# Four loads under way instead of three during the attention of a fused attention and two-MLP kernel, with the instruction orders rewritten to suit

## The chip, the core and the metric

The kernel runs on one core of one Trainium2 chip. A core has a matrix engine (PE; its weight loads are listed apart as PEld), a vector engine (DVE), a scalar engine (ACT), a general engine (POOL) and a sync engine (SP) that here only issues DMA transfers. Each engine works through its own list of instructions in order, and they wait for one another on semaphores. The metric is the time of the device for one execution in microseconds (us). The kernel before takes 612.75 us, the median of 3 runs (612.43 to 613.37).

## The reference

```
scores = scale * q @ k^T                 # q, k, v: 2 x 8 heads x 576 x 64, float32
mask: heads 0-3 local   (0 <= row - col < 32)
      heads 4-7 strided (col <= row, and row, col equal modulo 32)
x = softmax(scores) @ v                  # laid out as 1152 tokens x 512
h = max(x @ w_in, 0);  x = (h * h) @ w_out                       # 512 -> 2048 -> 512
p = domain_probs / (sum(domain_probs) + 1e-9)
out = sum over 4 experts e of p[:, e] * (max(x @ w1[e], 0) @ w2[e])   # 512 -> 1024 -> 512
```

## The kernel before

Every order in it is written out by hand, engine by engine.

**Attention.** The heads go in pairs, and a pair of one batch entry is a unit n = 0 to 7; units 0, 1, 4, 5 are local, the others strided. For each unit PE makes the scores (`scores(n)`: a mask product, L1313, and then the products of q and k, L1321), transposes the probabilities (`prob_transposes(n, h)`, L1334) and multiplies with v (`outputs(n)`, L1364). DVE takes the row maximum and subtracts it (`scores_max`, `scores_less`), ACT exponentiates (`exps`), DVE sums and inverts (`recip`), POOL multiplies (`normalised`, L621), ACT copies the transposed probabilities out of PSUM (`pT_copy`, L699) and then the result into `y` (`att_out`, L705). `keep_going` (L1370) gives PE idle products whose results nobody reads; `idle=` in a call says how many.

**First products.** The MLP products are done in a Strassen-like form with 7 products M1, M2, M6, M7, M4, M5, M3 in place of 8, each in three passes over a high and a low part of the numbers (L1374 to L1376). Their operands are made by `wa_high` (ACT, L717) and `wa_low` (POOL, L568) from the weights in `raw_a`; by `first_sum` (DVE) from sums of these; by `x_high` (ACT, L737) and `x_low` (POOL, L610, one of them on DVE, L955) from `y` or differences `t_form` of it; and by `wb_high` (ACT, L726) and `wb_low` from `raw_b`. `wa_high` of the first group waits until all four parts of `raw_a` are there, and the first `first_sum` too. `wb_high` waits for both parts of `raw_b`. M7 also needs `c_block(0, C11)` on DVE, which waits for the last `pT_copy`. The first of these products (block 0) lie between the last units of the attention, and after them PE goes through the rest of both MLPs.

**Loads.** SP issues them all, apart from half of one k. `load_qk(n)` is three transfers (q 288 KB, k 144 KB for each head) into one of three buffers, so it waits for `scores(n - 3)`. `load_v(n)` is 512 + 64 KB for a local unit and 384 KB for a strided one, and from n = 4 on waits for `outputs(n - 4)`. `load_a(0, parts)` brings 256 KB of weights for each part, `load_b(0, (i,))` 512 KB. Between loads stand `landed_qk(n)`, `landed_v(n)` and `landed_a(4)`, which hold SP until that load has landed, so that a fixed number of loads is under way.

Of the kernel before, what the change touches and what calls it, by code (L numbers as in the profile page):

```python
# [30 lines left out]
def attention_then_mlps(nc, qt, kt, v_near, v_last, v_far, wa, wb, probs, out):  # L31
# [60 lines left out]
    with ExitStack() as ctx:  # L92
# [313 lines left out]
        def _(sp):  # L406
# [58 lines left out]
            load_qk(2)  # L465
            landed_qk(0)
            load_a(0, (0, 1))
            landed_qk(1)
            load_v(0)
            landed_qk(2)  # L470
            load_a(0, (2, 3))
            load_qk(3)
            landed_v(0)
            load_v(1)
            landed_a(4)
            load_v(2)
            landed_qk(3)
            load_qk(4)
            landed_v(1)
            load_qk(5)  # L480
            landed_v(2)
            load_v(3)
            landed_qk(4)
            load_qk(6)
            landed_qk(5)
            load_qk(7)
            landed_v(3)
            load_v(4)
            landed_qk(6)
            load_v(7)  # L490
            landed_qk(7)
            load_v(5)
            landed_v(4)
            load_b(0, (0,))
            landed_v(7)
            load_v(6)
            landed_v(5)
# [19 lines left out]
        def _(pool):  # L517
# [109 lines left out]
            normalised(1)  # L627
            wa_low(0, A11)
            normalised(2)
            wa_low(0, A12)  # L630
            wa_low(0, S2)
            normalised(3)
            wa_low(0, S3)
            normalised(4)
            x_low(0, B11)
            normalised(5)
            x_low(0, B21)
            wa_low(0, A22)
            normalised(6)
            normalised(7)  # L640
# [3 lines left out]
            x_low(0, T1)  # L644
            x_low(0, B22)
            wa_low(0, S4)
            wb_low(0, 0)
            wb_low(0, 1)
            wb_low(0, 2)
            wb_low(0, 3)  # L650
            x_low(1, B11)
# [35 lines left out]
        def _(act):  # L687
# [86 lines left out]
            exps(1)  # L774
            pT_copy(0, 0)
            pT_copy(0, 1)
            exps(2)
            att_out(0)
            pT_copy(1, 0)
            pT_copy(1, 1)  # L780
            wa_high(0, A11)
            exps(3)
            wa_high(0, A12)
            pT_copy(2, 0)
            att_out(1)
            wa_high(0, S2)
            pT_copy(2, 1)
            x_high(0, B11)
            exps(4)
            wa_high(0, S3)  # L790
            att_out(2)
            pT_copy(3, 0)
            pT_copy(3, 1)
            wa_high(0, A22)
            exps(5)
            att_out(3)
            wa_high(0, S1)
# [3 lines left out]
            exps(6)  # L801
            pT_copy(5, 0)
            att_out(4)
            pT_copy(5, 1)
            exps(7)
            x_high(0, T2)
            first_product(0)
            att_out(5)
            x_high(0, T3)
            pT_copy(6, 0)  # L810
            pT_copy(6, 1)
            x_high(0, T4)
            pT_copy(7, 0)
            x_high(0, T1)
            pT_copy(7, 1)
            att_out(6)
            rectified(0, C11)
            wb_high(0, 0)
            x_high(0, B22)
            x_high(1, B11)  # L820
            wa_high(0, S4)
# [3 lines left out]
            rectified(0, C21)  # L825
            squared(0, C21)
            h_high(0, C21)
            wb_high(0, 2)
            wb_high(0, 3)
            rectified(0, C22)  # L830
            squared(0, C22)
# [746 lines left out]
```

## Time and profile before

| | us |
|---|---|
| median of 3 runs | 612.75 |
| profiled execution | 612.54 |
| its span in the trace | 610.7 |
| PE busy | 602.6 (99%) |
| DVE busy | 366.5 (60%) |
| POOL busy | 279.3 (46%) |
| ACT busy | 221.7 (36%) |

The span runs from the first to the last instruction; 1.84 us lie around it. PE is busy nearly throughout, but idle products count as busy too. In the chain that ended last, 94% of the span is PE, 3% DMA and 1% each SP's issues and DVE. In the span in 40 slices of 15.3 us, the DMA engines are busy 70% of the first slice, 90% of the second and 50% of the third, and 30% or less of each slice after that.

### The profile page before, as it was taken

To read this page: it belongs to the slowest core of one execution; us is meant where nothing else is said; L and a number is where in the kernel's file an instruction comes from. 1 tells how busy PE (TensorE), PEld (TensorE's weight loads), DVE (VectorE), ACT (ScalarE), POOL (GpSimd) and SP (SyncE) were. 2 spreads that over 40 slices of the span, in tenths; PEclk is the share of its full clock that TensorE was granted. 3 is DMA by queue.
4 is the path that set the end of the run, shared out by engine and by line. 5 is a ranking of instruction groups with operands and counts; after the bars stand their busy time and mean duration, and the time that the engine had idled before them with its cause. 6 is when DMAs were issued, how large, how long until landed. Compare 5 with 4: busy or idle time off the path is not lost.

```text
span 610.7 us, 11302 instructions
## 1 busy us (share of the span) xinstructions
PE 602.6 (99%) x4347; PEld 561.8 (92%) x4347; DVE 366.5 (60%) x797; ACT 221.7 (36%) x508; POOL 279.3 (46%) x230
## 2 busy tenths in 40 slices
PE   7899999999999999999999999999999999999998
PEld 6789999999999999998988989989989989989987
DVE  6787595746847878735636536636536446446452
ACT  2688373514524645511511421422332322232210
POOL 4679844551560587961560451462443353350300
PEclk9999999999999999999999999999999999999999
DMA  7953020220110220120220110220120030010012
GB/s 254 288 171 139 1 70 2 70 70 2 69 70 2 70 70 0 71 70 1 70 69 1 70 69 1 70 71 0 65 75 1 25 114 1 7 64 1 1 52 104
DMA packets 16677, 36.92 MB, mean 60 GB/s; under 512 B 2032, under 2 KB 2800, under 8 KB 16624
## 3 DMA queue, kind: packets, MB, share of 16 engines
q1 hardware_dynamic: 16544, 36.05, 17.3%
q8 instruction: 35, 0.57, 0.4%
q10 hardware_dynamic: 80, 0.15, 0.1%
q14 instruction: 18, 0.15, 0.1%
HBM read 33.84 MB, written 2.36 MB: 59 GB/s over the span
## 4 chain that ended last, share of the span: by engine, by line
PE 94%; DMA 3%; SPq 1%; DVE 1%; issue 0%; POOL 0%; ACT 0%; ACTq 0%
PE ps L1374 31%; PE ps L1376 31%; PE ps L1375 31%; DMA k_buf<-in_k 3%; PE ps L1364 1%; PE ps L1321 0%; DVE k_buf L1127 0%; PE ps L1334 0%; SPq L419 0%; SPq L412 0%; POOL prob L621 0%; SPq L438 0%; DVE ssum L919 0%; ACT y L705 0%; DVE t_form L944 0%
## 5 line engine op out<-in xcount | busy, mean ns | idle before, releaser
L1374 PE MATMUL ps<-xf_hi,wa_hi 128*128 128x288 f32 x672 | 199.3, 297 | 0.0
L1375 PE MATMUL ps<-xf_lo,wa_hi 128*128 128x288 f32 x672 | 198.3, 295 | 0.0
L1376 PE MATMUL ps<-xf_hi,wa_lo 128*128 128x288 f32 x672 | 197.6, 294 | 0.0
L574 POOL TENSOR_TENSOR wb_lo<-raw_b,wb_hi 128x512 fp32r<-128x512 f32 x48 | 61.0, 1307 | 175.9 <-ACT wb_hi L726 175.9
L1374 PEld LDWEIGHTS ps<-xf_hi,wa_hi 128*128 128x128 f32 x672 | 126.0, 187 | 0.9 <-ACT wa_hi L717 0.2
L1375 PEld LDWEIGHTS ps<-xf_lo,wa_hi 128*128 128x128 f32 x672 | 126.1, 188 | 0.5
L1376 PEld LDWEIGHTS ps<-xf_hi,wa_lo 128*128 128x128 f32 x672 | 126.5, 188 | 0.0
L1376 PE MATMUL ps<-wb_hi,h_lo 128*128 128x512 f32 (+1 forms) x292 | 113.0, 387 | 0.0
L1375 PE MATMUL ps<-wb_lo,h_hi 128*128 128x512 f32 (+1 forms) x292 | 113.0, 387 | 0.0
L1374 PE MATMUL ps<-wb_hi,h_hi 128*128 128x512 f32 (+1 forms) x292 | 112.8, 386 | 0.0
L1118 DVE SCALAR_TENSOR_TENSOR y<-ps,p_norm,y 128x512 f32<-128x512 f32 (+1 forms) x64 | 47.5, 742 | 102.3 <-PE ps L1376 102.3
L766 ACT ACTIVATE h_hi<-ps 128x288 fp32r<-128x288 f32 x128 | 50.5, 409 | 101.0 <-DVE ps L1077 100.8
L744 ACT ACTIVATE m<-ps 128x288 f32<-128x288 f32 x48 | 19.4, 413 | 183.7 <-PE ps L1376 183.7
L1374 PE MATMUL ps<-h_hi,wb_hi 128*128 128x288 f32 (+1 forms) x224 | 69.9, 312 | 0.0
L1376 PE MATMUL ps<-h_hi,wb_lo 128*128 128x288 f32 (+1 forms) x224 | 69.8, 312 | 0.0
L1375 PE MATMUL ps<-h_lo,wb_hi 128*128 128x288 f32 (+1 forms) x224 | 69.8, 311 | 0.0
L568 POOL TENSOR_TENSOR wa_lo<-raw_a,wa_hi 128x512 fp32r<-128x512 f32 x36 | 46.8, 1306 | 45.6 <-ACT wa_hi L717 45.6
L1077 DVE TENSOR_TENSOR ps<-ps,u 128x288 f32<-128x288 f32 x144 | 65.9, 459 | 2.0 <-PE ps L1376 0.3
L1376 PEld LDWEIGHTS ps<-wb_hi,h_lo 128*128 128x128 f32 x292 | 54.8, 188 | 11.1
L1375 PEld LDWEIGHTS ps<-wb_lo,h_hi 128*128 128x128 f32 x292 | 54.8, 188 | 10.9
L1374 PEld LDWEIGHTS ps<-wb_hi,h_hi 128*128 128x128 f32 x292 | 54.9, 188 | 10.8
L568 POOL TENSOR_TENSOR wa_lo<-s_form,wa_hi 128x512 fp32r<-128x512 f32 x48 | 61.3, 1296 | 7.6 <-ACT wa_hi L717 7.4
(88 smaller groups left out, 759.7 us busy)
## 6 DMA issues: line engine op xcount, KB each, us to landing
raw_a<-in_wa SPq DMA_DIRECT2D x48, 256.0 KB, 3.5
raw_b<-in_wb SPq DMA_DIRECT2D x24, 512.0 KB, 4.0
q_buf<-in_q SPq DMA_DIRECT2D x8, 288.0 KB, 4.4
k_buf<-in_k SPq DMA_DIRECT2D x15, 144.0 KB, 3.9
v_loc<-in_v_near SPq DMA_DIRECT2D x4, 512.0 KB, 4.3
result<-y SPq DMA_DIRECT2D x8, 256.0 KB, 2.0
v_str<-in_v_far SPq DMA_DIRECT2D x4, 384.0 KB, 4.4
v_loc<-in_v_last SPq DMA_DIRECT2D x4, 64.0 KB, 5.3
```

What stands on the lines that cost most here:

```text
L568: nc.gpsimd.tensor_tensor(wa_lo[:, k, :, :], where[:, i, :, :], wa_hi[:, k, :, :].bitcast(F32), ALU.subtract).then_inc(s_wa_lo, 1)
L574: nc.gpsimd.tensor_tensor(wb_lo[:, :, cols], raw_b[:, :, cols], wb_hi[:, :, cols].bitcast(F32), ALU.subtract).then_inc(s_wb_lo, 1)
L744: nc.scalar.activation(m1[:, u, :], ps[:, bank(t, M1, u), 0:HT], ACT.Copy).then_inc(s_m1, 1)
L766: nc.scalar.activation(dst, src, ACT.Relu).then_inc(s_h_hi, 1)
L1077: nc.vector.tensor_tensor(ps[:, hbank(t, q, u), 0:HT], ps[:, bank(t, k, u), 0:HT], other[:, u, :], ALU.add)\
L1118: nc.vector.scalar_tensor_tensor(out=out_acc[:, i, d], in0=src, scalar=p_norm[:, i, e:e + 1], in1=out_acc[:, i, d], op0=ALU.mult, op1=ALU. ...
L1364: ins = nc.tensor.matmul(dst, vals, probT[rows, n % 2, h, at:at + qw], start=True, stop=True)
L1374: nc.tensor.matmul(dst, a_hi, b_hi, start=first, stop=False)
L1375: nc.tensor.matmul(dst, a_hi, b_lo, start=False, stop=False)
L1376: return nc.tensor.matmul(dst, a_lo, b_hi, start=False, stop=last)
```

## The change

The order of the loads stays as it is. What moves is the wait before each: each stands one load later, so four loads are under way in place of three, and one wait (`landed_v(5)`) is gone. The orders of ACT, DVE, POOL and PE in the attention and the first MLP block are rewritten, and the idle products before `scores(4)` are gone. Nothing is computed otherwise. All lines behind the loads stand one line higher in the new file.

```
 sync:
             load_qk(2)
+            load_a(0, (0, 1))
             landed_qk(0)
-            load_a(0, (0, 1))
+            load_v(0)
             landed_qk(1)
-            load_v(0)
+            load_a(0, (2, 3))
             landed_qk(2)
-            load_a(0, (2, 3))
             load_qk(3)
+            load_v(1)
             landed_v(0)
-            load_v(1)
+            load_v(2)
             landed_a(4)
-            load_v(2)
+            load_qk(4)
...
 tensor:
             prob_transposes(0, 1)
-            outputs(0)
             prob_transposes(1, 0)
             prob_transposes(1, 1)
+            outputs(0)
             scores(3, idle=2)
             outputs(1)
             prob_transposes(2, 0)
             prob_transposes(2, 1)
-            scores(4, idle=3)
-            outputs(2)
+            scores(4)
             scores(5)
             prob_transposes(3, 0)
             prob_transposes(3, 1)
+            outputs(2)
             scores(6)
...
             product(0, M1, [1])
+            prob_transposes(6, 0)
+            prob_transposes(6, 1)
             outputs(5)
             product(0, M2, [0])
-            prob_transposes(6, 0)
-            prob_transposes(6, 1)
             product(0, M2, [1])
...
 gpsimd:
             normalised(1)
+            normalised(2)
             wa_low(0, A11)
-            normalised(2)
             wa_low(0, A12)
...
             x_low(0, T1)
+            wa_low(0, S4)
             x_low(0, B22)
-            wa_low(0, S4)
...
 vector:
             scores_max(1)
+            scores_less(1)
             recip(0)
-            scores_less(1)
+            recip(1)
             scores_max(2)
-            recip(1)
+            first_sum(S1)
             scores_less(2)
-            first_sum(S1)
+            first_sum(S3)
             recip(2)
+            first_sum(S2)
             pair_t1(0)
...
```

SP, from the loads of unit 4 on: the difference of the two orders. `v_str` and `v_loc` are v of strided and local units; `s_k_in0` to `s_k_in2` count landings in the three q and k buffers, `s_v_in0` to `s_v_in3` those of the v buffers, `s_pv` the finished `outputs`.

```order
-L431 DMA v_str<-in_v_far 128x768 [waits s_pv,s_k_in0,s_q_in0]
-L427 DMA v_loc<-in_v_near 128x2x512 [waits s_pv,s_k_in1,s_q_in1]
+L431 DMA v_str<-in_v_far 128x768 [waits s_pv,s_v_in3]
+L427 DMA v_loc<-in_v_near 128x2x512 [waits s_pv,s_k_in0,s_q_in0]
 L428 DMA v_loc<-in_v_last 64x2x128
-L445 DMA raw_b<-in_wb 128x1024 [waits s_v_in0]
-L431 DMA v_str<-in_v_far 128x768 [waits s_pv,s_v_in3]
-L445 DMA raw_b<-in_wb 128x1024 [waits s_v_in1]
+L445 DMA raw_b<-in_wb 128x1024 [waits s_k_in1,s_q_in1]
+L431 DMA v_str<-in_v_far 128x768 [waits s_pv,s_v_in0]
+L445 DMA raw_b<-in_wb 128x1024 [waits s_v_in3]
```

The second half of `raw_b` waited for v of unit 5, issued two transfers ahead of it; now it waits for v of unit 7, which is issued earlier still.

ACT at the start of the attention, from the first two `exps` (L691) on, before:

```order
4 L691 ACTIVATE raw_prob<-raw_prob 128x10x64 [waits s_less] x2
5 L699 ACTIVATE probT<-ps 128x320 [waits s_pT_ps] x2
6 L691 ACTIVATE raw_prob<-raw_prob 128x12x54 [waits s_less]
7 L705 ACTIVATE y<-ps 128x576 [waits s_pv]
8 L699 ACTIVATE probT<-ps 128x320 [waits s_pT_ps] x2
9 L717 ACTIVATE wa_hi<-raw_a 128x512 [waits s_raw_a]
```

and now (each line number is one lower):

```order
4 L690 ACTIVATE raw_prob<-raw_prob 128x10x64 [waits s_less] x2
5 L716 ACTIVATE wa_hi<-raw_a 128x512 [waits s_raw_a]
6 L698 ACTIVATE probT<-ps 128x320 [waits s_pT_ps]
7 L716 ACTIVATE wa_hi<-raw_a 128x512 [waits s_raw_a]
8 L698 ACTIVATE probT<-ps 128x320 [waits s_pT_ps]
9 L690 ACTIVATE raw_prob<-raw_prob 128x12x54 [waits s_less]
```

Two `wa_high`, with their wait for the weights, now stand ahead of the first and the second `pT_copy`, where one stood behind the fourth.

ACT around the last units, from `first_product` (L744, in the new file L743) on, before:

```order
35 L744 ACTIVATE m_62<-ps 128x288 [waits s_m] x2
36 L705 ACTIVATE y<-ps 128x576 [waits s_pv]
37 L737 ACTIVATE xf_hi<-t_form 128x576 [waits s_t0]
38 L699 ACTIVATE probT<-ps 128x384 [waits s_pT_ps,s_pv] x2
39 L737 ACTIVATE xf_hi<-t_form 128x576 [waits s_t0]
40 L699 ACTIVATE probT<-ps 128x384 [waits s_pT_ps,s_pv]
```

and now:

```order
36 L743 ACTIVATE m_62<-ps 128x288 [waits s_m] x2
37 L698 ACTIVATE probT<-ps 128x384 [waits s_pT_ps,s_pv] x2
38 L704 ACTIVATE y<-ps 128x576 [waits s_pv]
39 L725 ACTIVATE wb_hi<-raw_b 128x4x128 [waits s_raw_b]
40 L736 ACTIVATE xf_hi<-t_form 128x576 [waits s_t0] x2
41 L698 ACTIVATE probT<-ps 128x384 [waits s_pT_ps,s_pv] x2
```

The first `wb_high`, with its wait for both parts of `raw_b`, stood six rows further back; now it is ahead of the `x_high` of T3 and T4 and of the last two `pT_copy`.

## Rows read from the trace of the kernel before

**Rows 1.** PE over its first 52 us: start, length, engine, line, operation, count, [idle before <- releaser].
```profile
15.07 1.35 PE L1364 MATMUL ps<-probT,v_loc 64*64 64x32 f32 x72 [0.62 <-ACT probT L699]
...
16.99 0.71 PE L1370 MATMUL ps<-ones 128*128 128x512 f32 x2
...
17.94 1.26 PE L1321 MATMUL ps<-k_buf,q_buf 128*54 128x108 f32 x22
19.13 1.35 PE L1364 MATMUL ps<-probT,v_loc 64*64 64x32 f32 x72
21.03 0.85 PE L1334 MATMUL ps<-ident,prob 128*128 128x128 f32 x6 [0.54 <-POOL prob L621]
21.63 0.94 PE L1370 MATMUL ps<-ones 128*128 128x512 f32 x3
22.40 0.45 PE L1313 MATMUL ps<-mask_local,across 128*128 128x512 f32 x2
...
29.32 1.23 PE L1321 MATMUL ps<-k_buf,q_buf 128*54 128x108 f32 x22 [1.35 <-DMA k_buf<-in_k]
...
37.60 1.35 PE L1364 MATMUL ps<-probT,v_loc 64*64 64x32 f32 x72 [0.26 <-DMA v_loc<-in_v_last]
...
41.55 0.93 PE L1334 MATMUL ps<-ident,prob 128*128 128x128 f32 x6 [0.16 <-POOL prob L621]
...
50.77 0.30 PE L1374 MATMUL ps<-xf_hi,wa_hi 128*128 128x288 f32 x1
```
**Rows 2.** All waits of PE from 41 us to the end: us in total, times, longest.
```profile
PE ps L1334 <- POOL prob L621: 0.2, 1, 0.2
```
**Rows 3.** PE's granted clock, the span in 40 slices, in tenths (9 is 90% or more).
```profile
PEclk9999999999999999999999999999999999999999
```
**Rows 4.** The wait for the weights, seen on DVE (columns as in rows 1).
```profile
15.63 0.69 DVE L963 TENSOR_TENSOR s_form<-raw_a 128x512 f32<-128x512 f32 x1 [0.62 <-DMA raw_a<-in_wa]
```
**Rows 5.** SP's issues: start, length, line, transfer, count.
```profile
7.43 0.58 SPq L427 DMA_DIRECT2D v_loc<-in_v_near  x1
...
8.91 0.89 SPq L438 DMA_DIRECT2D raw_a<-in_wa  x2
...
31.48 0.33 SPq L431 DMA_DIRECT2D v_str<-in_v_far  x1
...
37.58 0.33 SPq L445 DMA_DIRECT2D raw_b<-in_wb  x1
```
**Rows 6.** Stretches: length, engines' busy us (count), PE clock, DMA share, GB/s.
```profile
8.00:10.50 2.50, 2.38 (x42) 1.87 (x41) 2.45 (x4) 0.74 (x1) 0.00 (x0) 1.00 0.67 199
10.50:29.00 18.50, 16.21 (x350) 13.52 (x349) 14.80 (x25) 10.85 (x22) 10.63 (x9) 1.00 0.94 298
28.00:29.00 1.00, 0.00 (x0) 0.00 (x0) 0.96 (x2) 1.00 (x3) 1.00 (x2) 1.00 0.93 195
32.50:40.50 8.00, 7.74 (x197) 7.33 (x198) 7.73 (x12) 6.02 (x14) 6.29 (x5) 1.00 0.88 291
```
**Rows 7.** ACT: columns as in rows 1.
```profile
21.64 0.61 ACT L717 ACTIVATE wa_hi<-raw_a 128x512 fp32r<-128x512 f32 x1
22.16 0.47 ACT L699 ACTIVATE probT<-ps 128x384 f32<-128x384 f32 x1
22.53 0.64 ACT L705 ACTIVATE y<-ps 128x576 f32<-128x576 f32 x1
...
40.30 0.69 ACT L737 ACTIVATE xf_hi<-t_form 128x576 fp32r<-128x576 f32 x1 [0.65 <-DVE t_form L944]
```
**Rows 8.** The chain that ended last: start, length, what.
```profile
23.65 5.53 DMA k_buf<-in_k
```
**Rows 9.** DMA issues between 37.5 and 37.9 us: count, KB each, us from issue to landing.
```profile
raw_b<-in_wb SPq DMA_DIRECT2D x1, 512.0 KB, 4.8
```
**Rows 10.** POOL: columns as in rows 1.
```profile
42.17 1.41 POOL L610 TENSOR_TENSOR xf_lo<-t_form,xf_hi 128x576 fp32r<-128x576 f32 x1 [0.76 <-DVE xf_lo L955]
...
48.97 1.29 POOL L568 TENSOR_TENSOR wa_lo<-s_form,wa_hi 128x512 fp32r<-128x512 f32 x1
```

More of the change, by code:

```diff
@@ L627, in _ @@
             normalised(1)
+            normalised(2)
             wa_low(0, A11)
-            normalised(2)
             wa_low(0, A12)
@@ L644, in _ @@
             x_low(0, T1)
+            wa_low(0, S4)
             x_low(0, B22)
-            wa_low(0, S4)
             wb_low(0, 0)
@@ L649, in _ @@
             wb_low(0, 2)
+            x_low(1, B11)
             wb_low(0, 3)
-            x_low(1, B11)
             x_low(1, B21)
@@ L774, in _ @@
             exps(1)
+            wa_high(0, A11)
             pT_copy(0, 0)
+            wa_high(0, A12)
             pT_copy(0, 1)
             exps(2)
+            pT_copy(1, 0)
             att_out(0)
-            pT_copy(1, 0)
+            wa_high(0, S2)
             pT_copy(1, 1)
-            wa_high(0, A11)
+            att_out(1)
             exps(3)
-            wa_high(0, A12)
             pT_copy(2, 0)
-            att_out(1)
-            wa_high(0, S2)
+            wa_high(0, S3)
             pT_copy(2, 1)
             x_high(0, B11)
+            wa_high(0, A22)
             exps(4)
-            wa_high(0, S3)
-            att_out(2)
             pT_copy(3, 0)
             pT_copy(3, 1)
-            wa_high(0, A22)
+            att_out(2)
             exps(5)
             att_out(3)
-            wa_high(0, S1)
             pT_copy(4, 0)
@@ L801, in _ @@
             exps(6)
+            x_high(0, T2)
+            att_out(4)
+            wa_high(0, S1)
             pT_copy(5, 0)
-            att_out(4)
             pT_copy(5, 1)
             exps(7)
-            x_high(0, T2)
             first_product(0)
-            att_out(5)
-            x_high(0, T3)
             pT_copy(6, 0)
             pT_copy(6, 1)
+            att_out(5)
+            wb_high(0, 0)
+            x_high(0, T3)
             x_high(0, T4)
             pT_copy(7, 0)
-            x_high(0, T1)
             pT_copy(7, 1)
             att_out(6)
+            x_high(0, T1)
             rectified(0, C11)
-            wb_high(0, 0)
+            wa_high(0, S4)
             x_high(0, B22)
             x_high(1, B11)
-            wa_high(0, S4)
             h_high(0, C11)
@@ L827, in _ @@
             h_high(0, C21)
+            x_high(1, B21)
             wb_high(0, 2)
-            wb_high(0, 3)
+            x_high(1, T2)
             rectified(0, C22)
             squared(0, C22)
-            x_high(1, B21)
+            wb_high(0, 3)
             h_high(0, C22)
@@ L836, in _ @@
             h_high(0, C12)
-            x_high(1, T2)
             x_high(1, T3)
@@ L1161, in _ @@
             recip(6)
+            t_forms(0, T4)
+            pair_t1(4)
             scores_less(7)
[L1163 to L1164 removed]
+            t_forms(0, T3)
             recip(7)
[L1166 removed]
             pair_t1(5)
@@ L1466, in _ @@
             prob_transposes(0, 1)
-            outputs(0)
             prob_transposes(1, 0)
             prob_transposes(1, 1)
+            outputs(0)
             scores(3, idle=2)
@@ L1473, in _ @@
             prob_transposes(2, 1)
-            scores(4, idle=3)
-            outputs(2)
+            scores(4)
             scores(5)
@@ L1478, in _ @@
             prob_transposes(3, 1)
+            outputs(2)
             scores(6)
```

72 lines of the change are left out of this document (34 added, 38 removed).

## The prediction

> **What bounds the kernel now.** I read the waits of PE first, since PE is busy 99% of the span. From 41 us to the end there is one wait, of 0.2 us [rows 2]. So 569 us of the span are PE's own work, the change touches none of it in length, and what it can bring is only how early PE gets there. Then I read PE's timeline up to that point [rows 1] for what is not needed work. It waits 0.62 us at 15.07 for ACT's copy of the transposed probabilities, 0.54 at 21.03 for POOL's probabilities, 1.35 at 29.32 for k of unit 6, 0.26 at 37.60 for v of unit 5 and 0.16 at 41.55 for POOL again. Between 21.63 and 22.40 it runs the three idle products ahead of `scores(4)`: 0.77 us. Third, what is behind the 1.35: k of unit 6 was issued at 23.65 and took 5.53 us [rows 8]. In the DMA engines' shares of the stretches [rows 6] the reader is to see that they are not idle in that time: 0.94 busy from 10.5 to 29 us, and only 0.67 from 8 to 10.5 us. A fourth load under way can fill 0.33 x 2.5 = 0.83 us of the one and 0.06 x 18.5 = 1.1 us of the other, 1.9 us in all.
>
> **The loads.** Nothing is added or removed but one wait; every load can be issued one landing earlier. The weights `raw_a`: their third and fourth part go out at 8.91 and about 9.35 [rows 5]; DVE is released by them at 15.63 after 0.62 us of waiting [rows 4]. The wait ahead of them is now that for unit 1, which was over at 7.43, where it released v of unit 0 [rows 5]; that load now goes out ahead of it. So they go out at about 7.6, some 1.25 us earlier. They can't land sooner by more than the idle share in front of them, 0.83 us; from below, they may gain nothing. I take nearly all of it, since that stretch is the emptiest: landing at 14.7 in place of 15.55 (between 14.3, the whole lead in issue, and 15.55).
>
> K of unit 6 can be issued once `scores(3)` is done. If the loads gain their whole 1.9 us, it lands at 29.18 - 1.9 = 27.3; with nothing, at 29.18.
>
> **The start of the attention: a loss.** ACT now waits for all of `raw_a` ahead of its first `pT_copy`. With R the landing, one `wa_high` takes 0.52 from start to next start, a `pT_copy` 0.37 and 0.47 to its end [rows 7]. The first copy starts at R + 0.52, the second `wa_high` at R + 0.89, the second copy at R + 1.41 and ends at R + 1.88. The second half of the transposes of unit 1 waits for that copy, takes half of 0.60 (from 21.03 to 21.63), and `outputs(0)` follows. Together `outputs(0)` and the transposes took 16.99 - 15.07 = 1.92; without the first half of the transposes, now done in the wait, 1.62. So PE has both behind it at R + 3.5 = 18.2, against 16.99: 1.2 us late, though both probabilities are ready sooner. `scores(3)` starts at 17.94 + 1.2 = 19.15.
>
> **From there to `scores(6)`: a gain.** In the run before these starts lie 29.32 - 17.94 = 11.38 us apart. Out of it go the idle products (0.77), the wait for `prob` with its small gap (21.03 - 19.13 - 1.29 = 0.6, taking 1.29 as the pitch of an `outputs` of 72 products, their 1.35 less the overlap) and the wait for k (1.35). The wait for `prob` goes because `normalised(2)` no longer has a `wa_low` of 1.29 us [rows 10] in front of it, and because transposes of unit 2 come later now. `outputs(2)` moves behind two `scores`, which gives its copies time. That leaves 8.65 us: `scores(6)` at 27.8 in place of 29.32, 1.5 us sooner. K of unit 6 has to be there by 27.8: 1.4 us of the 1.9 that the idle shares allow. `scores(3)` ends at about 20.4, the second half of k goes out within a microsecond of it, and even with the 5.53 us of before it lands at 26.9, so the buffer is not what holds it.
>
> **From `scores(6)` to the dense part.** The work is the same. The 0.26 and 0.16 may go: the transposes of unit 6 (0.6 us) now stand ahead of `outputs(5)`, which hides the landing of v, and `normalised(6)` no longer stands behind an `x_low`. Between 0 and 0.4; I take 0.2. Sum for PE: 1.7 us.
>
> **The end of the hand-over: raw_b.** ACT's first `wb_high` now stands ahead of `x_high` of T3 and T4, and it waits for the second half of `raw_b`. Before, that half went out at 37.58 [rows 5] and landed 4.8 us later [rows 9], at 42.4. POOL started on T3 at 42.17 and had the last operand of product M3 at 48.97 + 1.29 = 50.26 [rows 10]; M3 began at 50.77 [rows 1]. So POOL had 0.5 us to spare. Call the landing L: T3's `x_high` starts at L + 0.5 and takes 0.69 [rows 7], POOL starts at L + 1.2, and M3 can start at L + 1.2 + (50.26 - 42.17) = L + 9.3. To be 1.7 us sooner M3 needs L of 39.8 or less. Now that half waits for v of unit 7, which was issued at 31.48 [rows 5] as soon as `outputs(3)` was done, 1.6 us sooner now: 29.9. The DMA engines moved 291 GB/s at 0.88 from 32.5 to 40.5 [rows 6] for v7, v5, b0, v6 and b1; at 0.94 that is 7.5 us. With 1.0 us from issue to first bytes (31.48 to 32.5) and a tail of 0 to 1.9 us (40.5 to 42.4): L between 38.4 and 40.3. So this costs 0 to 0.5 us; I take 0.2. Were it to land as late as before, it would cost 2.6 us.
>
> **Sum.** +1.2 -0.77 -0.6 -1.35 -0.2 +0.2 = -1.5 us. Profiled execution: 612.54 - 1.5 = 611.0; it stands 0.2 under the median of the three runs, 612.75, so I predict 612.75 - 1.5 = 611.2. A change of 0.2% (1.2 us, to 611.5 or 614.0) is about the least that these runs tell from none.
>
> **A rule against it.** In the last microsecond of the wait for k, 28 to 29, the DMA engines are 0.93 busy and move only 195 GB/s, where the stretch as a whole moves 298 at 0.94 [rows 6]: busy engines, fewer bytes. The Trainium skill says in "DMA: Bandwidth & Descriptors", section "Latency and other measured facts", that the latency of HBM access is the larger part of a DMA's fixed cost and grows with load. By that rule a fourth load would stretch the other three, and the idle shares would fill without bytes. The trace agrees in this one stretch and not in the others.
>
> **Rivals.**
> (a) *The loads land no sooner*, because the engines that carry them are full and only the queue in front of them grows. For it: 0.94 busy, and the 195 GB/s. Against it: the 0.67 from 8 to 10.5. Then R = 15.55, `scores(3)` starts at 20.0 and PE would reach `scores(6)` at 28.65; k is there at 29.18. Gain 0.1 at that point, 0 to 0.4 with the later waits: 612.5. With `raw_a` alone late it would be 0.7 + 0.2 = 0.9: 611.9.
> (b) *raw_b holds ACT.* Mechanism as above; each microsecond of L after 39.8 moves M3 by one. It turns slower than before at L = 50.77 - 9.3 = 41.5, and slower by 0.2% at 42.7, about where it landed before (42.4: 613.6). For it: the 4.8 us for a load with little else under way [rows 9]. Against it: its issue comes about 4 us earlier. It would need a landing 9 us after its issue. Price at 43: 614.3.
> (c) *More is gained*: `raw_a` lands at 14.3 and the dense part is reached with all of 0.4 us gone, L not binding: -2.3, 610.4.
> (d) *PE's clock falls* in the new waits, of 1 us or so between 14.3 and 16.6. For it: fewer idle products. Against it: the 1.35 us wait left the granted clock as it was [rows 1, 3]. 3 us at 1.2 in place of 2.4 GHz would cost 1.5: 612.7.
>
> **Chances.** Forecast (a gain of 1.0 to 2.0) 0.46; (c) 0.12; (a) in both its forms 0.28; (b) slower than before 0.10; (d) 0.04. Faster by over 0.2% needs a gain of 1.25: some 0.38 of the first 0.46 and all of (c), 0.50. Slower by over 0.2%: 0.07, from (b) and what I have not seen. Within: 0.43. The range holds (a), the forecast and most of (c): 610.0 to 612.9. The forecast's own is 610.7 to 611.7.
>
> **What would show it.** ACT idle for the weights ahead of the first `pT_copy`, its first `wa_high` starting at 14.3 to 15; `outputs(0)` at 16.9 and `scores(3)` at 19.1, later than before; no wait for `prob` in unit 2 and none above 0.3 us for k of unit 6, `scores(6)` at 27.4 to 28.3; the last transposes at 39.6 to 40.1 in place of 41.55; ACT's first `wb_high` at 39 to 40.3 and M3 at 49.0 to 49.6. DMA share from 10.5 to 27 us of 0.97 with more than 298 GB/s would be the deeper queue at work; the same GB/s at a higher share would be (a). The prediction is wrong if the 569 us behind 41.55 change by more than 0.5 us, since I count them as fixed, or if `scores(3)` is not late at all, for then ACT's order costs nothing and the gain is above 2.

## The result: 0.4% slower, where 0.2% faster was forecast

The changed kernel takes 615.07 us, the median of 17 runs (612.39 to 617.44); the kernel before took 612.17 beside it, the median of 17 (610.84 to 613.47). The ratio is 1.0044, 95% interval 1.0031 to 1.0057: 2.9 us slower. The forecast was 1.5 us faster, 611.2, and its range ended at 612.9. In 8 of the 17 runs PE's granted clock over the whole run was a little under 1.00. The 9 others have a mean of 613.81; all 17 have one of 614.95. One run of the kernel before (880.16 us, beside e5 to e8) and one of e15 (655.84) fell into a slower state of the chip; they are in no ratio, count or mean below.

The profiled execution took 615.94 us, its span 614.2 against 610.7. PE's clock fell in it, so its 3.5 us hold that too, and no execution of the changed kernel with a full clock was profiled. PE up to the last product that the change touches (start, length, engine, line, operation, count, [idle before <- releaser]):

```profile
13.48 0.85 PE L1333 MATMUL ps<-ident,prob 128*128 128x128 f32 x6
16.57 0.55 PE L1333 MATMUL ps<-ident,prob 128*128 128x128 f32 x3 [2.24 <-ACT probT L698]
17.41 0.55 PE L1333 MATMUL ps<-ident,prob 128*128 128x128 f32 x3 [0.30 <-ACT probT L698]
17.89 1.47 PE L1363 MATMUL ps<-probT,v_loc 64*64 64x32 f32 x72
19.30 1.22 PE L1369 MATMUL ps<-ones 128*128 128x512 f32 x2
...
20.99 1.92 PE L1320 MATMUL ps<-k_buf,q_buf 128*54 128x108 f32 x22
...
30.62 1.26 PE L1320 MATMUL ps<-k_buf,q_buf 128*54 128x108 f32 x22
...
42.70 0.71 PE L1333 MATMUL ps<-ident,prob 128*128 128x128 f32 x5
43.64 0.33 PE L1333 MATMUL ps<-ident,prob 128*128 128x128 f32 x1 [0.23 <-issue]
...
47.84 0.37 PE L1373 MATMUL ps<-xf_hi,wa_hi 128*128 128x288 f32 x1 [1.25 <-DVE ps L1076]
...
49.96 0.91 PE L1363 MATMUL ps<-probT,v_str 64*64 64x54 f32 x44 [0.29 <-DVE t_form L1017]
...
54.27 0.37 PE L1373 MATMUL ps<-xf_hi,wa_hi 128*128 128x288 f32 x1
```

Against [rows 1] these are, in order: `outputs(0)` done at 19.30 in place of 16.99 (+2.3), `scores(3)` at 20.99 in place of 17.94 (+3.05), `scores(6)` at 30.62 in place of 29.32 (+1.3), the last transposes at 42.70 in place of 41.55 (+1.15), and M3 at 54.27 in place of 50.77 (+3.5). So there are two losses, one at the start (part of it the clock's) and one behind 42.70, and the gain forecast between `scores(3)` and `scores(6)` lies between them. The reader is to see the two releasers: `probT`, which ACT copies late at the start, and `ps L1076`, which DVE computes late at the end. Both lead back to ACT, which stood before a load (DVE stood before the same load at the start, see e2):

```profile
15.56 0.63 ACT L716 ACTIVATE wa_hi<-raw_a 128x512 fp32r<-128x512 f32 x1 [3.86 <-DMA raw_a<-in_wa]
16.10 0.42 ACT L698 ACTIVATE probT<-ps 128x320 f32<-128x320 f32 x1
...
44.66 0.63 ACT L725 ACTIVATE wb_hi<-raw_b 128x512 fp32r<-128x512 f32 x1 [2.90 <-DMA raw_b<-in_wb]
45.20 1.24 ACT L736 ACTIVATE xf_hi<-t_form 128x576 fp32r<-128x576 f32 x2
46.35 0.85 ACT L698 ACTIVATE probT<-ps 128x384 f32<-128x384 f32 x2
```

The two loads in the chain that ended last (start, length, what). The first `wb_high` starts 8.5 us after the issue of its load, which took 4.8 us before [rows 9]:

```profile
8.81 6.72 DMA raw_a<-in_wa
...
36.13 8.51 DMA raw_b<-in_wb
```

SP's issues show why that load was not sooner: v of unit 7 goes out at 32.80, where [rows 5] had 31.48 and the prediction 29.9.

```profile
8.23 1.01 SPq L438 DMA_DIRECT2D raw_a<-in_wa  x2
...
32.80 0.33 SPq L431 DMA_DIRECT2D v_str<-in_v_far  x1
...
35.07 0.54 SPq L445 DMA_DIRECT2D raw_b<-in_wb  x1
35.70 0.38 SPq L431 DMA_DIRECT2D v_str<-in_v_far  x1
36.13 0.42 SPq L445 DMA_DIRECT2D raw_b<-in_wb  x1
```

The stretches of [rows 6] again (length, busy us of PE, PEld, DVE, ACT, POOL with counts, PE clock, DMA share, GB/s), and the one in which the clock fell:

```profile
8.00:10.50 2.50, 2.38 (x41) 1.93 (x41) 2.43 (x4) 0.74 (x1) 0.00 (x0) 1.00 0.90 204
10.50:29.00 18.50, 15.71 (x300) 12.75 (x299) 12.56 (x22) 8.83 (x18) 10.02 (x8) 0.91 0.86 287
...
32.50:40.50 8.00, 7.75 (x192) 6.97 (x186) 7.71 (x14) 6.69 (x16) 6.31 (x4) 1.00 0.76 219
...
19.00:22.50 3.50, 3.50 (x34) 2.90 (x30) 1.14 (x3) 1.50 (x3) 3.29 (x3) 0.51 0.97 330
```

From 8 to 10.5 us the engines' share rose from 0.67 to 0.90 and the bytes from 199 to 204 GB/s: nearly a quarter of the stretch more in use, and almost nothing more moved (how much this scatters is at the end). A clock of 0.51 over 3.5 us, 1.2 in place of 2.4 GHz, lost about 1.7 us of full-speed time in this execution.

### The profile page after: what moved, and what is told of

Its sections match the earlier page's. It is cut to its first block, busy times and chain, and to the rows that moved or that the text cites. A ratio compares the mean times of both kernels' runs of the same rounds, so it can differ in the third digit from the quotient of the medians.

```text
span 614.2 us, 11297 instructions
## 1 busy us (share of the span) xinstructions
PE 604.7 (98%) x4344; PEld 562.5 (92%) x4344; DVE 365.0 (59%) x797; ACT 221.6 (36%) x508; POOL 280.3 (46%) x230
## 3 DMA queue, kind: packets, MB, share of 16 engines
HBM read 33.84 MB, written 2.36 MB: 59 GB/s over the span
## 4 chain that ended last, share of the span: by engine, by line
PE 93%; DMA 2%; SPq 1%; DVE 1%; ACT 1%; issue 0%; POOL 0%; DVEq 0%; ACTq 0%
PE ps L1373 31%; PE ps L1375 30%; PE ps L1374 30%; DMA raw_b<-in_wb 1%; DMA raw_a<-in_wa 1%; PE ps L1363 1%; PE ps L1320 0%; DVE k_buf L1126 0%; SPq L427 0%; POOL prob L620 0%; SPq L438 0%; ACT probT L698 0%; PE ps L1333 0%; SPq L419 0%; ACT xf_hi L736 0%
## 5 line engine op out<-in xcount | busy, mean ns | idle before, releaser
L743 ACT ACTIVATE m<-ps 128x288 f32<-128x288 f32 x48 | 19.5, 413 | 184.6 <-PE ps L1375 184.6
L1076 DVE TENSOR_TENSOR ps<-ps,u 128x288 f32<-128x288 f32 x144 | 65.8, 459 | 1.6
```

Of the source, the lines that this page charges most:

```text
L743: nc.scalar.activation(m1[:, u, :], ps[:, bank(t, M1, u), 0:HT], ACT.Copy).then_inc(s_m1, 1)
L1076: nc.vector.tensor_tensor(ps[:, hbank(t, q, u), 0:HT], ps[:, bank(t, k, u), 0:HT], other[:, u, :], ALU.add)\
```

## The experiments

Each kernel was timed beside the kernel before, in five rounds except e13. "Clock 1.00" is the mean of the runs whose granted clock was 1.00, with their number; scatter between such runs is 0.5 to 1.1 us, so a mean of 8 is good to some 0.35. That of the kernel before was 612.36 beside e1 to e4, 612.39 beside e5 to e8, 612.95 beside e9 to e12 and 612.45 beside e13 to e15 (beside the change, where its clocks were not kept, the mean of all 17 was 612.04). So kernels of different groups are to be compared by their distance from it.

| kernel | median | ratio to before, 95% | clock 1.00 |
|---|---|---|---|
| the change | 615.07 | 1.0044, 1.0031 to 1.0057 | 613.81 (9 of 17) |
| e1 `wb_high` back | 612.23 | 1.0010, 0.9992 to 1.0028 | 612.02 (8 of 12) |
| e14 `raw_b` loaded early | 612.85 | 1.0022, 1.0000 to 1.0045 | 612.43 (7 of 12) |
| e2 `wa_high` back | 614.13 | 1.0035, 1.0019 to 1.0051 | 613.83 (8 of 12) |
| e8 `raw_a` counted apart, and e1 | 612.62 | 1.0003, 0.9990 to 1.0016 | 612.25 (6 of 11) |
| e6 idle products behind the wait | 617.96 | 1.0089, 1.0071 to 1.0107 | 617.49 (2 of 6) |
| e9 idle products in the wait | 613.58 | 1.0019, 1.0002 to 1.0037 | 614.02 (10 of 12) |
| e3 three loads, new orders | 615.53 | 1.0053, 1.0033 to 1.0073 | 614.46 (2 of 7) |
| e5 e1 and e2 together | 612.77 | 1.0008, 0.9997 to 1.0020 | 612.56 (7 of 12) |
| e10 e5 with three loads | 613.23 | 1.0013, 0.9997 to 1.0030 | 612.93 (7 of 12) |
| e4 four loads, old orders | 611.62 | 0.9993, 0.9980 to 1.0005 | 612.03 (12 of 12) |
| e7 e4, last load held | 611.26 | 0.9985, 0.9975 to 0.9994 | 611.53 (11 of 11) |
| e12 e5, last load held | 612.11 | 0.9992, 0.9980 to 1.0005 | 612.18 (11 of 12) |
| e11 e7 without idle products | 611.91 | 0.9984, 0.9971 to 0.9997 | 612.01 (11 of 12) |
| e15 e4, `raw_b` early, no idle | 611.57 | 0.9983, 0.9969 to 0.9997 | 611.70 (11 of 11) |

**e1_wb_back: is it the wait for raw_b?** The changed kernel with the first `wb_high` back behind `rectified(0, C11)`.

```
             att_out(5)
-            wb_high(0, 0)
             x_high(0, T3)
...
             rectified(0, C11)
+            wb_high(0, 0)
```

> The changed kernel, with ACT's first wb_high back behind rectified(0, C11), where it stood before. Theory 1 (ACT's wait for raw_b ahead of the last transposed copies is a loss): ACT no longer idles 2.9 us near 42 us, PE's wait for DVE's c_block (1.2 us) goes, and the time falls by about 2 us against the changed kernel, to 613. Theory 2 (the clock's fall in the first wait is all of the loss): no change, 615, and runs with a granted clock under 1.0 stay as frequent. Theory 3 (the deeper queue itself is the loss): no change, 615.

At clock 1.00 it takes 1.8 us less than the changed kernel. The waits behind 42 us are gone, and the start is as it was, with its wait and its fall of the clock (PE and ACT, then the stretch 19 to 23 us):

```profile
16.29 0.55 PE L1333 MATMUL ps<-ident,prob 128*128 128x128 f32 x3 [2.10 <-ACT probT L698]
...
42.40 0.82 PE L1333 MATMUL ps<-ident,prob 128*128 128x128 f32 x6
...
47.38 0.91 PE L1363 MATMUL ps<-probT,v_str 64*64 64x54 f32 x44
...
15.28 0.63 ACT L716 ACTIVATE wa_hi<-raw_a 128x512 fp32r<-128x512 f32 x1 [3.72 <-DMA raw_a<-in_wa]
...
19.00:23.00 4.00, 4.00 (x64) 3.30 (x62) 1.19 (x3) 1.50 (x3) 4.00 (x4) 0.64 0.93 343
```

`outputs(7)` stands at 47.38 in place of 49.96. At clock 1.00 this one row of ACT's order is all of the loss that can be told; 4 of 12 runs still had a lower clock.

**e14_b_early: is it the landing, or the place in the order?** The changed kernel, orders untouched, with the two halves of `raw_b` right behind v of units 4 and 5.

```
             load_v(4)
+            load_b(0, (0,))
...
             load_v(5)
+            load_b(0, (1,))
             landed_qk(7)
-            load_b(0, (0,))
...
             landed_v(7)
-            load_b(0, (1,))
```

> The changed kernel with raw_b's first half issued right behind v of unit 4 and its second half right behind v of unit 5, so that neither waits for v of unit 7 to land. If the landing of raw_b is what holds ACT at its first wb_high, that wait of 2.9 us falls under 1, and the time comes down from 613.8 (full clock) by 1 to 2 us, to that of the kernel with wb_high moved back, 612.0. If it is wb_high's place that costs and not the landing, no change.

Issued at 28.64 and 32.92, both halves are there when ACT comes to `wb_high` at 40.41:

```profile
40.41 0.62 ACT L725 ACTIVATE wb_hi<-raw_b 128x512 fp32r<-128x512 f32 x1
```

It has no wait, and clock 1.00 gives 612.43 in place of 613.81, level with the kernel before (612.45). So at clock 1.00 this place in ACT's order is harmless once the load is early; what was wrong was the landing that I gave it. 5 of 12 runs had a lower clock still.

This execution also began otherwise: its first scores took 2.36 us where those of the change took 1.29, though the granted clock stands at 1.00 there.

```profile
6.60 2.36 PE L1320 MATMUL ps<-k_buf,q_buf 128*32 128x128 f32 x36 [0.48 <-DMA k_buf<-in_k]
```

The same holds for the profiled executions of e8, e11 and e12 (2.35 to 2.36). They come to the first transposes up to 3 us late, when the weights have nearly landed or are there, so they say little on what an edit did to the waits at the start.

**e2_wa_back: what does the wait at the start cost by itself?** `wa_high` A11 and A12 moved behind `att_out(0)`, `wb_high` left where the change has it.

```
-            wa_high(0, A11)
             pT_copy(0, 0)
-            wa_high(0, A12)
...
             att_out(0)
+            wa_high(0, A11)
+            wa_high(0, A12)
```

> The changed kernel, with ACT's first two wa_high moved behind att_out(0), so that the copies of the transposed probabilities of unit 0 don't wait for raw_a. Theory 1a (this wait is a loss of 1.2 to 2.5 us for PE): PE's wait of 2.2 us at 16.6 falls under 0.7, no run has a granted clock under 1.0, scores(6) starts 1.5 to 3 us sooner, and the time falls by 1 to 2.5 us, to 613 to 614. Theory 1b (only the wait for raw_b counts, which ends with the loads): 615 still. Theory 2 (the clock): no clock under 1.0, and the time of the runs with a full clock stays at 614.

Nothing at clock 1.00: 613.83 against 613.81. PE's waits (us in total, times, longest) show two things that I had not thought of: a wait of 2.1 us for the copies of unit 1, and 1.7 us in which it waits for nothing that the trace shows.

```profile
PE ps L1363 <- ACT probT L698: 2.1, 1, 2.1
...
PE ps L1333 <- issue: 1.0, 1, 1.0
...
PE ps L1312 <- issue: 0.7, 1, 0.7
```

The wait of 2.1 us comes from DVE. The new order puts `first_sum(S1)`, which waits for `raw_a`, ahead of `scores_less(2)`, where it stood behind it. So DVE holds `exps(2)` on ACT, and the second copy of unit 1 comes only after that and after three `wa_high`, the first of them at 18.53, long after the weights:

```profile
15.55 0.69 DVE L962 TENSOR_TENSOR s_form<-raw_a 128x512 f32<-128x512 f32 x1 [2.46 <-DMA raw_a<-in_wa]
...
17.02 0.75 ACT L690 ACTIVATE raw_prob<-raw_prob 128x648 f32<-128x648 f32 x1 [2.66 <-DVE raw_prob L911]
...
20.09 0.43 ACT L698 ACTIVATE probT<-ps 128x320 f32<-128x320 f32 x1
```

No experiment puts this third wait back. The end of the hand-over follows the landing of `raw_b` (ACT at 44.95, 3.45 us of waiting), so what happens at the start is hidden. It is not evidence that the start is free. 4 of 12 runs still had a lower clock; in the profiled one it fell to 0.53 from 21 to 22 us, right behind the wait of 2.1 us.

**e8_own_sem: e1 with the first two parts of raw_a counted on a semaphore of their own**, so that `wa_high` A11 and A12 need not wait for parts 2 and 3.

```
-    sp.dma_start(raw_a[:, i, :, :], ...).then_inc(s_raw_a, 16)
+    sp.dma_start(raw_a[:, i, :, :], ...).then_inc(s_raw_a01 if s == 0 and i < 2 else s_raw_a, 16)
...
+    if s == 0:
+        act.wait_ge(s_raw_a01, 32)
```

> The changed kernel with wb_high back in its old place, and with the first two parts of raw_a counted on a semaphore of their own, so that ACT's first two wa_high wait for these alone (landing at about 11.5) and not for all four (15.4). ACT then has no wait of 3.7 us, PE's of 2.1 us falls under 0.5 and no run has a granted clock under 1.0. If PE's delay at the start is worth something once raw_b holds nothing, the time is 610.5 to 611.5; if not, 612.

In the profile ACT has no wait for the weights, but this execution is one of those with late first scores, and that of e1 had a fall of the clock, so the two traces (`outputs(7)` at 46.20 against 47.38) are no fair pair. At clock 1.00 it is 612.25 against 612.02: no difference that can be told. Letting ACT's first two `wa_high` go ahead brings nothing measurable in time while the clock holds; 5 of 11 runs had a lower clock even so.

**e6_idle_start and e9_idle_in_wait: is it the idleness that drops the clock?** e6 gives the first half of the transposes of unit 1 fourteen idle products; e9 puts ten between the transposes of units 0 and 1.

```
 e6:
-            prob_transposes(1, 0)
+            prob_transposes(1, 0, idle=14)
 e9:
             prob_transposes(0, 1)
+            keep_going(10, OBANK)
             prob_transposes(1, 0)
```

> The changed kernel with 14 idle products (14 x 0.21 = 3.0 us) in PE's wait for the first transposed copy. If the granted clock falls because PE waits there for 2.2 us, no run has a clock under 1.0, and the time is that of the changed kernel's runs at full clock, 613.8, up to 0.8 more where the products outlast the wait. If the clock falls for another reason, half of the runs still have 0.997 or less and the median stays at 615.

> The changed kernel with 10 idle products (2.1 us) between the transposes of unit 0 and those of unit 1, so that they run inside PE's wait for the first transposed copy; the 14 of the run before stood behind that wait and so only added to it. If the clock falls because PE stands still there for 2.2 us, no run has a granted clock under 1.0 and the median falls from 615 to the 613.8 of the changed kernel's runs at full clock. If it falls for another reason, about half of the runs still have under 1.0.

In e6 the products stood behind PE's wait and not in it, a mistake in the experiment, and they only made PE later (this row, and one that I come back to):

```profile
17.15 3.49 PE L1369 MATMUL ps<-ones 128*128 128x512 f32 x14 [2.36 <-ACT probT L698]
...
45.55 0.29 PE L1375 MATMUL ps<-xf_hi,wa_lo 128*128 128x288 f32 x1 [1.80 <-issue]
```

Yet this execution is of use: behind a wait of 2.36 us, with the idle products right after it, the granted clock stayed at 1.00 to 30 us. It fell later, to 0.50 from 47 to 49 us, behind the stall of 1.80 us of the second row.

In e9 they do lie in the wait. The clock was under 1.00 in 2 of 12 runs in place of 8 of 17, and the ratio is 1.0019 in place of 1.0044. Against the kernel before in the same comparison e9 is 1.1 us slower at clock 1.00 (614.02 and 612.95), the change 1.8. So e9 had fewer falls, which cost the change about 1.1 us on the mean (614.95 - 613.81), but 2 of 12 against 8 of 17 can still be chance, and how much of its gain is theirs is not told apart. That a wait of 2 us is needed for a fall is not so: the profiled execution of e9 was one of the two that fell, behind a wait of 1.23 us.

```profile
13.94 2.56 PE L1369 MATMUL ps<-ones 128*128 128x512 f32 x10
17.73 0.55 PE L1333 MATMUL ps<-ident,prob 128*128 128x128 f32 x3 [1.23 <-ACT probT L698]
...
19.00:23.00 4.00, 4.00 (x80) 3.35 (x80) 2.07 (x4) 1.98 (x5) 2.62 (x2) 0.53 0.88 272
```

**e3_three_loads and e4_before_four: the loads and the orders apart.** e3 is the changed kernel with SP's list of before, e4 the kernel before with SP's new list (the `sync` part of the diff above, undone and done alone).

> The changed kernel with SP's list of before: three loads under way, the new orders of all other engines kept. Theory 1 (the orders are the loss, and the loads land no sooner with four): raw_a lands at 15.5 as well, raw_b some microseconds later, at 42 to 47, and the time is 615 to 617. Theory 3 (four under way is the loss): 612 to 613.

> The kernel before with four loads under way and nothing else changed. If the loads land sooner with four under way, the wait of 1.35 us for k of unit 6 shrinks and the time falls by up to 1.4 us, to 611. If the queue only gets longer (theory 1), each load lands within 0.5 us of where it did and the time is within 0.5 us of before, 612.2. Theory 3 (the deeper queue is the loss of the change): 614 to 615.

e3 is as slow as the change: `raw_b` goes out at 41.69, ACT waits 2.0 us for it and starts at 45.77. The new orders alone bring the loss, whatever the number of loads. e4 is not slower than before, and its own trace says that the fourth load did bring what [rows 8] promised, and where it went (PE):

```profile
27.55 1.26 PE L1320 MATMUL ps<-k_buf,q_buf 128*54 128x108 f32 x22
...
40.02 0.41 PE L1333 MATMUL ps<-ident,prob 128*128 128x128 f32 x2
41.89 0.64 PE L1333 MATMUL ps<-ident,prob 128*128 128x128 f32 x4 [1.47 <-issue]
...
46.70 0.91 PE L1363 MATMUL ps<-probT,v_str 64*64 64x54 f32 x44
```

`scores(6)` is at 27.55 in place of 29.32, 1.8 us sooner with the idle products still in, since the wait for k is gone. Then PE stands still for 1.47 us in the middle of six transposes of one group, with all operands there, and the gain is spent: `outputs(7)` at 46.70 against 46.64 before.

**e5_both_back, e10_new_three: the new orders without either of ACT's two waits.** Both edits of e1 and e2; e10 also has three loads.

```
 e5:  wb_high(0, 0) as in e1, wa_high(0, A11) and wa_high(0, A12) as in e2
 e10: e5, and the sync list of the kernel before
```

> The changed kernel with both of ACT's waits for loads put back: the first wb_high behind rectified(0, C11), the first two wa_high behind att_out(0). If the two waits are the whole loss and the rest of the change is a gain, this is faster than with wb_high alone moved back (612.0 at full clock): PE's 2.1 us wait at the start now counts, some 611. If the wait at the start was only covering for a later one (the loads from v of unit 6 on), it stays at 612.

> The new orders with ACT's two waits for loads put back and three loads under way, as before. With four under way this stood at 612.6, and PE stood still once for 1.2 us in the middle of a mask product with nothing missing. Theory A (PE's own instructions come late behind four loads): no such stall; the time is that of four under way or up to 1 us better if the loads land as soon, 611.5 to 612.6. Theory B (the loads need the fourth): PE waits again for k of unit 6, 613 or more.

Neither differs from before by what can be told (612.56 against 612.39 and 612.93 against 612.95 at clock 1.00). The new orders with ACT's two waits removed are worth nothing. DVE's wait for `raw_a` is still in them (1.24 us in e5, 1.65 in e10), and behind it PE waits 0.72 and 1.30 us for the copies of unit 1. In both PE stands still ahead of the second mask product, e5 first, then e10 with three loads, where it does so twice:

```profile
25.04 0.46 PE L1312 MATMUL ps<-mask_local,across 128*128 128x512 f32 x2 [1.22 <-issue]
```
```profile
25.43 0.45 PE L1313 MATMUL ps<-mask_local,across 128*128 128x512 f32 x2 [1.18 <-issue]
...
42.51 0.33 PE L1334 MATMUL ps<-ident,prob 128*128 128x128 f32 x1 [0.53 <-issue]
```

My theory until e10 was that the deeper queue of loads caused the stall. It falls in that form: three loads show it too.

**e7_four_b1_late, e12_new_b1_late: one load held back.** e4 and e5 with the wait that the change dropped kept ahead of the second half of `raw_b`.

```
             landed_v(7)
+            landed_v(5)
             load_b(0, (1,))
```

> The kernel before with four loads under way, but the second half of raw_b held until v of unit 5 has landed, as in the kernel before. In the kernel before with four loads PE reached the transposes of unit 7 at 40.0 in place of 41.55 and then stood still for 1.5 us between two of their matmuls with no data missing. If its own instructions came late because they queue behind the loads, the longest queue (raw_b and v of unit 6) is shorter here, the stall goes, and the time is 1 to 1.5 us under before, 611. If the stall has another cause it stays, and so does 612.

> The new orders with ACT's two waits put back, four loads under way, and the second half of raw_b held for v of unit 5. If late instructions of PE are what keeps these orders at 612.6, the stall at 24 us is untouched by this (its queue is that of q, k and v) and the time stays near 612.5; if raw_b's half had a part in it, 611.5.

e7 is faster than before: 0.9985, 0.9975 to 0.9994, a gain of 0.9 us. Its transposes of unit 7 run through, and `outputs(7)` stands at 45.26:

```profile
40.13 0.97 PE L1334 MATMUL ps<-ident,prob 128*128 128x128 f32 x6 [0.33 <-POOL prob L621]
```

Against e4 it is 0.5 us at clock 1.00, not 1.5, so the stall is not in each execution of e4, or is not always as long. e12 has no stall in its profile either. Set against before in its own comparison it is 0.8 us faster at clock 1.00, where e5 is 0.2 slower; the ratio (0.9980 to 1.0005) does not quite tell it from before, nor from e7. So holding this load is a gain with either orders, as far as can be told, and the new orders add nothing to it.

**e13_shift: do the stalls go with a count of instructions?** e5 with 40 idle products of 128 columns in place of 10 of 512 (the same columns, 30 matmuls more ahead of the first stall; they took 2.45 us for each twenty in place of 1.45 for five); one execution, profiled.

```
-                keep_going(idle, TBANK + h)
+                small_steps(4 * idle, TBANK + h)
```

> The new orders with ACT's two waits put back and four loads under way, with the two times five idle products of 512 columns ahead of the first transposes written as two times twenty of 128 columns: the same 1.1 us each, but 30 matmuls more. In three profiles of such orders PE stood still behind its 344th matmul of the trace, at the second mask product of scores(5) with nothing missing. If its instructions come in blocks, and late, the stall stays behind about the 344th matmul and so moves up in the program, into the products of scores(4). If it is a wait for data or for another engine, it stays at scores(5), now behind the 374th matmul.

There was no stall at all in it (612.4 us, span 610.6), and its first transposes began 2 us later than those of e5. By itself it decides nothing; the last section has what it says together with the others.

**e11_late_no_idle, e15_best: what else in the change was worth taking.** e11 is e7 without the idle products ahead of `scores(4)`; e15 is the kernel before with four loads, `raw_b` early as in e14, and those idle products gone.

```
-            scores(4, idle=3)
+            scores(4)
```

> The kernel before with four loads under way, the second half of raw_b held for v of unit 5, and without the three idle products ahead of scores(4). With them it took 611.5. PE no longer waits for k of unit 6 there, so the 0.77 us of these products may be on the path: 610.8 if all of it is, 611.5 if ACT, DVE and POOL set the pace of the next units.

> The engine orders of before, the loads four under way with raw_b early as in the run above, and without the three idle products ahead of scores(4). With raw_b's second half late this took 611.5 to 612.0, against 612.4 to 613 of before in the same rounds. If the longer queue ahead of v of unit 5 and 6 costs nothing, 611.5 again; if PE waits for v of unit 5 or its own instructions, 612.5.

Without the 0.77 us of idle products PE waits as long for others, here e11's two longest of these:

```profile
24.07 0.84 PE L1334 MATMUL ps<-ident,prob 128*128 128x128 f32 x6 [0.54 <-POOL prob L621]
...
27.27 0.91 PE L1364 MATMUL ps<-probT,v_str 64*64 64x54 f32 x44 [0.82 <-ACT probT L699]
```

They stood in time that PE did not have. e15 gives 0.9983 (0.9969 to 0.9997), e7 0.9985: both beat both kernels, and are not told from one another.

## Why the prediction was wrong

**The step that failed** is "The end of the hand-over: raw_b", its term "L between 38.4 and 40.3. So this costs 0 to 0.5 us; I take 0.2." L was 44.65 in the profiled execution, 4.3 us behind the upper end; in the end time the term measured 1.4 us (e14) to 1.8 us (e1) at clock 1.00, or 1.8 to 2.1 by the distances from before. The mechanism was rival (b)'s, and its formula held: M3 at L + 9.3 = 53.95, measured 54.27. Its chance, 0.10, was too small. Two inputs of L were wrong. Issue: v of unit 7 waits for `outputs(3)`, and I let that be 1.6 us sooner with the rest, while all before it was 1.3 us late (32.80 in place of 31.48, against 29.9). The clock's fall ahead of it, 1.7 us, is in that; at a full clock L would have been sooner by up to as much, which is an estimate. The gain at the end was used to price an edge that hung on it. Flight: I took the 291 GB/s of before and scaled them up to a share of 0.94; the engines moved 219 GB/s at a share of 0.76 there, and the load took 8.5 us. I had written that it "would need a landing 9 us after its issue" as if that spoke against it. With five loads issued within 3.8 us, each one took longer than the one ahead of it: 3.1, 4.7, 6.3, 7.7 and 8.5 us.

**The sum, term by term.** From the starts of the profiled execution: `scores(3)` +3.05 (forecast +1.2), from there to `scores(6)` -1.75 (-2.7), to the last transposes -0.15 (-0.2), to M3 +2.35 (+0.2), together +3.5 for -1.5. About 1.7 us of the first two are the clock's. The prediction's own sign of being wrong came too: it counted the 569 us behind 41.55 as fixed, and they are 571.5 (614.2 - 42.70).

**The start: mechanism right, size wrong.** "Landing at 14.7 in place of 15.55": it was 15.56. The issue was earlier (8.23 in place of 8.91, not 7.6, since the two issues of v ahead of it take 1.2 us of SP), and all of that was lost in flight: rival (a). The Trainium skill's sentence in "DMA: Bandwidth & Descriptors", section "Latency and other measured facts", that the latency of HBM access grows with load, pointed the same way, and here the trace agrees: the last part took 6.4 us from issue to landing, 5.7 before. One execution is not the rule, though: DVE was released by these weights at 15.03 to 15.28 in e1, e4, e5 and e7 and at 15.55 in e2, with four loads, and at 15.46, 15.63 and 15.96 in e10, before and e3, with three. R + 3.5 gives 19.06 for `outputs(0)` done; measured 19.30. By itself this loss is not seen in the end time at clock 1.00 (e8 and e5 against e1).

**A wait that the prediction did not name.** It had two waits for loads that moved forward, both on ACT. There is a third, DVE's in `first_sum(S1)` ahead of `scores_less(2)` (2.02 us in the change, 2.46 in e2). In the change it ends with ACT's own and so hides behind it.

**The clock: a rival with too small a chance.** (d) had 0.04. The clock fell in 8 of 17 runs, some 1.1 us on the mean. What I held against it, the 1.35 us wait of [rows 1] that left the clock alone [rows 3], was a shorter wait; this one is 2.24 us. All 17 profiled executions together speak for the longer wait. The clock fell behind waits of 2.24 us (the change), 2.10 (e1), 2.11 (e2) and 2.62 (e3), behind e6's stall of 1.80, and once behind a shorter one (e9, 1.23). It did not in the 11 whose longest wait after 8 us was 1.47 or less, nor behind e6's 2.36 with idle products right after it. But that is one execution of each, and it is not settled: e5 and e8 had 5 of 12 and 5 of 11 runs below 1.00, though their profiled executions waited 1.22 us at most, while the kernel before had 1 of 30, 2 of 28, 5 of 35 and 2 of 23. With the old orders and four loads it was 0 of 12 (e4), 0 of 11 (e7), 1 of 12 (e11) and 0 of 11 (e15), with the new ones 4 to 5 of 11 or 12 in e1, e2, e5, e8, e10 and e14, but 1 of 12 in e12, which has the new orders and the last load held.

**The gain in the middle: right where it could be read, and worth little.** `scores(3)` to `scores(6)` took 9.63 us against a forecast of 8.65; 0.66 of the difference is `scores(3)` at half clock (1.92 in place of 1.26), 0.24 a wait for POOL. In e4 `scores(6)` comes 1.8 us sooner, which is the wait for k with something over. I counted each of these microseconds as one of the end time. They were not: the idle products stood in slack (e11), and the next thing to be late was not on my list, PE without instructions to run. In e7, whose profile has no such stall, 0.9 us reached the end time.

**Right:** the 564 us behind `outputs(7)` are fixed, 564.06 us before (610.7 - 46.64) and 564.24 after (614.2 - 49.96), 564.1 to 564.3 in the experiments.

**Open:** why e5 and e8 are not faster than before at clock 1.00, though `outputs(7)` comes 0.8 and 0.4 us sooner in their profiles; what DVE's wait for `raw_a` costs; why the clock falls more often with the new orders; and what makes an execution of e4 or e5 stall.

## What to carry to other kernels

When an instruction with a load behind it is moved forward in an engine's queue, price it at the load's landing with everything issued just ahead of it still under way, not at bytes over bandwidth, and check whether the issue itself hangs on the gain that you are adding up. A load issued earlier into busy DMA engines may land little sooner than it did; to get it sooner something must stand behind it (e14), not merely beside it. Look for such waits on every engine whose order changes, not on one alone. Change the number of loads under way and the orders in separate steps: e7, the change's list of loads with one wait kept and none of its orders, gains the 0.15% that the whole change lost three times over.

## What the runs showed that was not expected

**PE stands still with nothing missing, at set counts of its own instructions.** The stalls marked "issue" come after 344 matmuls (e2, e5, e10), 595 (e14, 0.53 us) or 715 to 717 (the change, e2, e4, e10, e6), though these are different places of the program: a mask product, the products with v, the last transposes, and in e6 the middle of M2, inside which no matmul waits for a semaphore. Counted from the start of the span to within each stall (matmuls in the first brackets), e5, e4 and e6 in turn:

```profile
0.00:24.90 24.90, 20.41 (x344) 16.12 (x345) 17.29 (x31) 10.60 (x20) 14.11 (x26) 1.00 0.86 285
```
```profile
0.00:41.50 41.50, 36.60 (x715) 30.75 (x716) 32.20 (x52) 22.78 (x45) 26.28 (x35) 1.00 0.81 262
```
```profile
0.00:45.40 45.40, 38.44 (x717) 31.52 (x718) 30.57 (x52) 21.60 (x43) 26.51 (x34) 1.00 0.75 239
```

The page of the changed kernel has a DMA queue for instructions (packets, MB, share of 16 engines):

```profile
q8 instruction: 35, 0.57, 0.4%
```

0.57 MB in 35 packets is 16 KB each. PE runs 4344 matmuls and as many weight loads, 8688 instructions, which is 248 for each of the 35, so these packets are most likely PE's program. From 344 to 715 are 371 pairs, 742 instructions, about three packets' worth. In e4 one starts at about 39.5 and PE goes on at 41.89, 2.4 us later; in e5 the two are 22.75 and 25.04, in e6 43.25 and 45.55. Looked at in steps of 0.25 us, all nine stalls end 2.3 to 2.8 us after the start of such a packet. Where there was no stall, PE came to its 716th matmul 3.0 to 3.9 us after the packet (before, e1, e7, e12). And the later the packet starts in PE's own count, the longer the stall: at matmul 700 it is 0.23 us (the change), at 703 0.53 (e10), at 705 1.04 (e2), at 712 1.47 (e4), at 715 1.80 (e6), and at 696 or earlier none (e7, before, e1, e12). In e13 the packet starts at 20.75 and PE reaches 344 only past 24, so no stall was due. That PE waits for this packet is therefore well supported. The Trainium skill, "Runtime: NRT & Kernel Launch", section "Instruction fetch mechanics", says that instructions are refilled by DMA in 16 KiB blocks and that crossing a block is mostly hidden: the size agrees, and "mostly hidden" does not hold here, with stalls of 0.23 to 1.8 us. Why the packet starts late is not shown: that it queues behind the loads is argued from e7 and e12, and three loads stall as well (e10).

**The engines' share is no measure of room.** The idle 0.33 of the DMA engines from 8 to 10.5 us was the basis of a term of 0.83 us. It is not a property of three loads: there the share was 0.67 in the kernel before, 0.88 in e10 and 1.01 in e3, with 199, 240 and 209 GB/s, and with four it was 0.64 in e5, 0.84 in e7, 0.86 in e4 and 0.90 in the change, with 205, 244, 185 and 204. One execution gave me an idle share that the next did not have, and neither number follows the other. In e4 the second half of `raw_b` was issued 3.7 us sooner than before (33.90 against 37.58) and landed 0.4 us sooner, 42.0 against 42.4.
